# A fused attention and two-MLP kernel: clusters' ones transposed after the next group of weightings, guard maxima reduced ahead of the remainders, the third head's similarity moved to the first head's end

## The reference, cut to what matters

```python
B, H, S, D = 2, 8, 768, 64            # 16 heads in all, 16 clusters per head
q_assign = argmax(q_n @ c_n.T)        # the nearest centroid of each query ...
k_assign = argmax(k_n @ c_n.T)        # ... and of each key
mask = q_assign[..., :, None] == k_assign[..., None, :]
scores = where(mask, (q @ k.T) / sqrt(D), -1e9)
attn = exp(scores - max(scores)) / sum(...)
x = (attn @ v)                        # heads side by side: 1536 x 512
x = moe1(x)                           # 512 -> 2048 -> 512, leaky relu
out = moe2(x)                         # 512 -> 2048 -> 512, a rational function
```

## Time and profile before

| | |
|---|---|
| median of 3 runs | 825.64 us (824.8 to 826.27) |
| the profiled execution's own time | 822.96 us |
| its span | 821.2 us |
| PE busy | 791.4 us, 96% of the span |
| DVE, ACT, POOL busy | 562.2 (68%), 492.6 (60%), 296.1 us (36%) |
| chain that ended last | PE 77%, ACT 8%, DVE 6%, issue 5% |

### The profile page before, as it was taken

The page is one execution under the profiler, slowest core; times in us unless marked ns, Lnnn a source line. Parts: engine busy times, 40 slices in busy tenths (PEclk is TensorE's granted clock), DMA queues, the critical chain, the costliest instruction groups (busy, mean ns, idle before and its releaser), DMA issues.

```text
span 821.2 us, 13189 instructions
## 1 busy us (share of the span) xinstructions
PE 791.4 (96%) x4339; PEld 747.0 (91%) x4339; DVE 562.2 (68%) x948; ACT 492.6 (60%) x836; POOL 296.1 (36%) x330
## 2 busy tenths in 40 slices
PE   6799999999999999999999999979999999999996
PEld 5589999999999999999999999969988998998994
DVE  5777877877874555433433454488888888888885
ACT  2367777877887111211211233479999999999995
POOL 7467988987985796000000036640000000000000
PEclk9999999999999999999999999989999999999999
DMA  7445654564442333000000024410001001001001
GB/s 201 115 110 137 160 154 123 147 168 117 110 100 72 97 102 105 0 0 0 0 0 0 0 76 122 124 40 1 1 0 38 0 0 38 0 0 39 1 1 38
DMA packets 30316, 52.15 MB, mean 64 GB/s; under 512 B 9184, under 2 KB 11328, under 8 KB 30272
## 3 DMA queue, kind: packets, MB, share of 16 engines
q1 hardware_dynamic: 30272, 51.59, 22.9%
HBM read 29.40 MB, written 3.19 MB: 40 GB/s over the span
## 4 chain that ended last, share of the span: by engine, by line
PE 77%; ACT 8%; DVE 6%; issue 5%; POOL 2%; DMA 1%; SPq 1%; POOLq 0%; ACTq 0%; DVEq 0%
PE ps L193 29%; PE ps L1011 16%; PE ps L1019 13%; PE ps L635 3%; PE ps L697 3%; PE ps L667 3%; PE ps L678 3%; PE ps L705 3%; PE ps L698 3%; PE ps L608 2%; ACT ps L787 1%; DMA sums<-scratch 1%; ACT scratch L1063 1%; ACT scratch L1069 1%; PE ps L622 1%
## 5 line engine op out<-in xcount | busy, mean ns | idle before, releaser
L199 ACT ACTIVATE g_hi<-g_f 128x384 fp32r<-128x384 f32 x128 | 67.4, 527 | 218.5 <-PE ps L1011 201.3
L211 DVE TENSOR_SCALAR corr<-ps,alpha_c 128x384 f32<-128x384 f32 x64 | 39.5, 617 | 130.3 <-PE ps L193 130.2
L193 PE MATMUL ps<-x_lo,w_hi_b 128*128 (+1 forms) x352 | 118.8, 337 | 0.0
L193 PE MATMUL ps<-x_hi,w_hi_b 128*128 (+1 forms) x352 | 118.7, 337 | 0.0
L193 PE MATMUL ps<-x_hi,w_lo_b 128*128 (+1 forms) x352 | 118.7, 337 | 0.0
L893 DVE TENSOR_REDUCE row_max<-ps 128x1 fp32r<-128x768 f32 x96 | 91.0, 950 | 35.4 <-PE ps L635 35.0
L784 ACT ACTIVATE probs_hi<-ps 128x768 fp32r<-128x768 f32 x96 | 78.1, 814 | 61.7 <-PE ps L678 60.9
L203 DVE TENSOR_TENSOR g_lo<-g_f,g_hi 128x384 fp32r<-128x384 f32 x128 | 82.2, 642 | 0.6 <-ACT g_hi L199 0.6
L340 DVE TENSOR_TENSOR probs_lo<-ps,probs_hi 128x768 fp32r<-128x768 f32 x64 | 61.0, 954 | 24.4 <-ACT ps L787 24.4
L340 POOL TENSOR_TENSOR probs_lo<-probs,probs_hi 128x768 fp32r<-128x768 f32 x32 | 59.6, 1862 | 47.4 <-ACT probs L787 47.4
L1159 POOL TENSOR_TENSOR w_lo_a<-stage,w_hi_a 128x512 f32 (+1 forms) x10 | 12.7, 1297 | 163.6 <-ACT w_hi_a L1084 163.6
(11 more groups left out here) (132 smaller groups left out, 2094.6 us busy)
## 6 DMA issues: line engine op xcount, KB each, us to landing
stage<-in_moe_w_in SPq DMA_DIRECT2D x27, 256.0 KB, 2.6
stage<-in_moe_w_out SPq DMA_DIRECT2D x27, 256.0 KB, 2.8
raw<-in_qk SPq DMA_DIRECT2D x16, 384.0 KB, 3.8
op_a<-head_hi SPq DMA_DIRECT2D x32, 192.0 KB, 3.4
v_raw<-in_v SPq DMA_DIRECT2D x16, 192.0 KB, 2.5
op_b<-head_hi SPq DMA_DIRECT2D x16, 192.0 KB, 3.5
op_b<-head_lo SPq DMA_DIRECT2D x16, 192.0 KB, 3.7
scratch<-spread SPq DMA_DIRECT2D x16, 192.0 KB, 4.1
```

The source lines that it names most:

```text
L193: last = pe.matmul(h_ps[j % H_RING][:, 0:BLK], a[:, 0, w], x[:, kt, cols], start=(kt == 0 and i == 0), stop=(kt == KT - 1 and i == 2))
L199: act.activation(g_hi[:, j % 2], g_f[:, j % 2], ACT.Copy).then_inc(g_hi_made, 1)
```

## The change

It makes four edits, with the waits and places on ACT and DVE that go with them.

1. `turn_onehot(n+2)` stands in slot 0 of head n (n >= 1), behind `weigh_hi` and ahead of the guards and the score, where before the same transposes stood at the end of slot 5 of the head before. `put_mask_k` follows `exp` of slot 0 in place of `exp` of the slot before it.
2. Ahead of the loop, one tile of `sim(2)` stands in front of `turn_first_max`, two behind guard 5, and the last one behind `score(0)`; guards 4 and 5 follow `turn_first_max` directly.
3. `sim(3)` moves from slot 1 to slot 4 of head 0, ahead of guard and score, and into banks 0 and 1; its reading on DVE moves with it, and `turn_onehot(2)` no longer waits for it.
4. DVE reduces all guards of a slot ahead of the remainder in the first seven slots too.

```diff
--- before.py
+++ after.py
@@ -278,7 +278,7 @@
 
 
 
-            SIM_BANK = {1: 7, 2: 4, 3: 7}
+            SIM_BANK = {1: 7, 2: 4}
 
             def sim_at(m, t):
                 if m in SIM_BANK:
@@ -598,11 +598,8 @@
                     if m == 2:
                         pe.wait_ge(mask_q_put, 1)
                         pe.wait_ge(mask_k_put, 1)
-                    if m == 3:
-                        pe.wait_ge(mask_q_put, 2)
-                        pe.wait_ge(mask_k_put, 2)
-                    if m >= 4:
-                        pe.wait_ge(guard_taken, T * (m - 1) - 2)
+                    if m >= 3:
+                        pe.wait_ge(guard_taken, T * (m - 1) - (1 if m == 3 else 2))
                         pe.wait_ge(sim_taken, m)
                     for t in tiles:
                         last = pe.matmul(sim_at(m, t), raw[:, m % 2, t * P:(t + 1) * P], cent_t[:, head_of(m)],
@@ -614,8 +611,6 @@
                     pe.wait_ge(onehot_made, m + 1)
                     at_least(pe, mask_q_put, m)
                     at_least(pe, mask_k_put, m)
-                    if m == 2:
-                        pe.wait_ge(sim_taken, 4)
                     if m >= 3:
                         pe.wait_ge(pv_taken, 2 * (m - 3) + 1)
                     for t in range(T):
@@ -729,26 +724,29 @@
                 sim(2, range(0, 2))
                 guard(0, 2)
                 guard(0, 3)
+                sim(2, range(2, 3))
                 turn_first_max()
-                sim(2, range(2, 4))
                 guard(0, 4)
-                sim(2, range(4, T))
                 guard(0, 5)
+                sim(2, range(3, 5))
                 turn_max(0)
                 for g in range(UNITS + LAG):
                     n, s = g // U, g % U
                     if g >= LAG:
                         weigh_hi(g - LAG)
                     if g < UNITS:
+                        if g == U - 2:
+                            sim(3)
                         if g == U - 1:
                             turn_max(1)
+                        if s == 0 and n >= 1 and n + 2 < N:
+                            turn_onehot(n + 2)
                         guards(n, s, 1)
                         scores_free(g)
                         score(g)
                         if g == 0:
+                            sim(2, range(5, T))
                             turn_onehot(1)
-                        if g == 1:
-                            sim(3)
                         if n >= 1 and s == 1 and n + 3 < N:
                             sim(n + 3)
                         if n >= 1 and s == 3 and n + 1 < N:
@@ -764,8 +762,6 @@
                         guards(n, s, 3)
                         if g == 2:
                             turn_onehot(2)
-                        if s == U - 1 and n + 3 < N:
-                            turn_onehot(n + 3)
 
 
             @block.scalar
@@ -819,8 +815,8 @@
                     exp(g)
                     if n == 0 and s in (0, 2):
                         put_mask_k(1 + s // 2)
-                    if s == U - 1 and n + 3 < N:
-                        put_mask_k(n + 3)
+                    if n >= 1 and s == 0 and n + 2 < N:
+                        put_mask_k(n + 2)
                     if s == 2 and n >= 1:
                         take_pv(n - 1, 1)
                     if s == 4:
@@ -932,23 +928,17 @@
                     if s == (5 if n == 0 else 3) and n + 1 < N:
                         take_max(n + 1)
 
-                    late = n == 0 or (n, s) == (1, 0)
-                    for m, t in guard_tiles(n, s, *((1, 2) if late else (1, 2, 3))):
+                    for m, t in guard_tiles(n, s, 1, 2, 3):
                         take_guard(m, t)
-                    if n >= 1 and s == 1 and n + 3 < N:
+                    if g == U - 2 or n >= 1 and s == 1 and n + 3 < N:
                         nearest(n + 3)
-                    if n == 0 and s == 3:
+                    if g == 3:
                         put_mask_q(2)
                     if n >= 1 and s == 0 and n + 2 < N:
                         put_mask_q(n + 2)
                     if s not in POOL_LO:
                         make_lo(dve, g)
-                    if g == 1:
-                        nearest(3)
-                    if late:
-                        for m, t in guard_tiles(n, s, 3):
-                            take_guard(m, t)
-                    if n == 0 and s == 2 or n >= 1 and s == 3 and n + 3 < N:
+                    if g == U - 2 or n >= 1 and s == 3 and n + 3 < N:
                         ranked(n + 3)
                         first_nearest(n + 3)
                     if s == 4 and n % 2 == 0 and n >= 2:
```

## The result

The changed kernel takes 818.9 us (median of 4 runs, 816.96 to 819.34), the kernel before beside it 825.38: a ratio of 0.9916 [0.9898, 0.9934], a gain of 6.9 us (5.4 to 8.4); the two medians lie 6.5 us apart. Forecast were 820.7 us and a gain of 4.9: the direction and the range held, the gain was forecast too small. The profiled execution of the change took 819.34 us, 817.5 of it span; that of before 822.96. This pair is only 3.6 us apart, less than the 4.9 forecast, and its attention ends 3.6 us earlier too (the last matmul starts at 263.82 for 267.42).

The account below looks back on a forecast made before the run. PE, busy 96% of the span, was taken as the bound, so only its idle or low-clock time can be won. Transposes 2.2 plus start 2.7 make 4.9 us: 825.64 - 4.9 = 820.7 us, range 818.6 to 824.2.

Parts of the forecast that it names:

- Part 1: Transposes one group of weightings later, behind `weigh_hi`: 2.34 us of PE's waits less 0.1 that stays, 2.2 us gained.
- Part 2: The start's new order laid end to end: scores of slot 7 from 49.93 to 47.25, 2.7 us gained.
- link 6: `sim(3)` in slot 4 of head 0: needs the eleventh reduction (35.6), costs 1.33 us; 3.1 us of lead left.
- 5, guard of 36.48: Reduction of place 3 ahead of `make_lo`: the guard at 36.48 starts at 32.2, 4.3 us ahead.
- 7, guard of 45.08: End of head 0, DVE's chain after `exp`: guard starts at 42.65, 2.4 us ahead, PE idle some 1.8 us.
- link 2: First scores go from 23.58 to 22.15; if the DMA issued at 19.07 lands late, 1.4 us are lost.
- link 4: Head 1's guards: POOL ends at 27.25, DVE is through `ranked(2)` by 27.7; second guard 31.71 to 28.65, 3.05 us.
- The sum: 2.2 + 2.7 = 4.9 us: 820.7 against the 825.64 median, 818.1 for the profiled execution; MLPs' work untouched.
- Only one part shows: The transposes' gap is its own price, or DVE eats the start's lead: 823.4 or 822.9 us; chance 0.14.
- DVE held beside POOL: Slot 3, DVE loses 1.5 us: six heads cost 5.1, 825.8 us (chance 0.04); twelve 10.2, 830.9; slower 0.04.
- The clock rises at another time: PE reaches 2.4 GHz later in the start, 1.5 us lost, 822.2; or earlier, 0.8 won, 819.9; chance 0.08.
- It does not do what it says: Transposes still wait because POOL's ones set the pace; waits stay and the start gives little, chance 0.04.

Follow-up runs that it names:

- e8: The change with three tiny memsets on DVE ahead of `ranked` from head 4 on, so DVE starts behind POOL; 823.86 us, 0.9994 to the kernel before.

## Why the prediction was right or wrong

**What bounds the kernel: right.** PE's busy time did not move (791.4 to 790.8 us), and what the profiles show as won is time in which PE had stood still or run at its lower level.

**Part 1 (2.2 us): right.** Reading the waits off PE's own distances, not off the view of waits (5.4), gave the size: 2.08 us in the profile, 1.7 in the two others of the change, 1.80 in that of edit 1 alone, 2.6 (1.6 to 3.5) timed. On top of edits 2 to 4 it shows less: the ratio goes from 0.9944 to 0.9937 and to 0.9925, 0.6 and 1.6 us. That ACT's later mask copy would cost nothing held: the heads are 14.69 us apart, 0.02 above the 14.67 of a head without a wait. The waits for ACT's copy of the output come and go: none in the change's profile, 0.2 and 0.3 us in its two others, 0.3 with edit 1 alone, where 0.1 was kept.

**Part 2, link by link: right in the profile.** (The forecast of link 6 is the 40.12 of that guard before, less the 3.1 us left.)

| link | forecast | change's profile |
|---|---|---|
| 1, `turn_max(0)` | 21.5 | 21.82 |
| 2, first scores | 22.15 | 22.45 |
| 3, second scores | 24.95 | 25.07 |
| 4, head 1's second guard | 28.65 | 28.96 |
| 5, guard of 36.48 | 32.2 | 32.49 |
| 6, guard behind `sim(3)` | 37.0 | 37.13 |
| 7, guard of 45.08 | 42.65 | 42.83 |
| 8, scores of slot 7 | 47.25 | 47.38 |

The late DMA that link 2 feared did not hold ACT: the wait ahead of the first scores is the 0.36 us it was. In link 4 `ranked(2)` was held beside POOL again, 1.50 us, since it starts 0.44 us behind POOL. The Trainium skill (SBUF — State Buffer, Who interferes with whom), drawn on there for which of the two blocks the other, agrees in this place: DVE began second and was held. It does not describe, where DVE began second too and was not held; the last section has that.

**The sum: the step that failed.** The term "So part 2 gives 2.7 us" is too small for the kernel. It is right for the start of slot 7 in the profiled pair, 2.55, but edits 2 to 4 alone give 4.6 us timed (3.5 to 5.7), twice. The prediction saw that the profiled execution of before lay 2.7 us below the median, and then took the same 4.9 us off the median, as if what makes an ordinary execution longer lay outside the change. Part of it lies inside. The averages of the profiled executions show how much:

| | slot 7 starts | attention's last matmul starts |
|---|---|---|
| before (six) | 50.5 | 268.2 |
| edit 1 alone (one) | 50.0 | 265.7 |
| edits 2 to 4 alone (two) | 46.9 | 264.1 |
| the change (three) | 47.7 | 264.0 |

So the profiles give edits 2 to 4 4.1 us, inside the timed interval and 1.4 above the term. About 0.5 of the 1.4 is the clock: in two of six executions of before it rose late, in the very microseconds that edits 2 to 4 rearrange, and that costs before 1.6 us, the new start 0.3 (e8). In before the twelve matmuls of `sim(3)` stand in those microseconds and take 2.74 us in place of 1.50, with the guard that DVE needs next behind them; in the new order they come later, at 35.8. Another 0.5 us are won between slot 7 and the attention's end (217.7 us on average before, 217.2 with edits 2 to 4 alone), where part 2 was put at nothing; which waits these are was not traced. The last 0.4 is within what slot 7 moves by from one execution to the next. The clock was a rival, but only for the kernel after; that the kernel before has two starts was not asked.

**What stays open.** How often the clock rises late is not known: two of six executions of before, and one (e8) of the eight that hold the whole new start, are too few to say whether the new order changes it. The profiled executions of before average 823.6 us (six, four of them on another chip), those timed beside the other kernels 825.0 (52 executions). One place where a longer execution can get its time is the second slow stretch between the MLPs, 1.4 us, seen in four of the twelve profiles of changed kernels and in none of before; whether the timed executions of before have it, no profile shows.

**Why the parts don't add up.** 2.6 + 4.6 = 7.2 us, while the whole gave 6.9, 5.2 and 6.2. Averaged over all executions (16 of the change, 819.45 us; 52 of before, 824.95, other runs and chips among them) it is 5.5 us (4.7 to 6.3 by their scatter). The profiles have the gap too: 2.5 + 4.1 against 4.2 us by the attention's end. Of these 2.4, 0.7 is that slot 7 starts later in the three of the change, one of which was held up by a DMA, and 0.6 the new wait of 0.9 us in head 13, in two of three. The rest is open, and the new wait was not taken away by itself. So 4.9 lies 0.6 us under the mean over all executions, inside its scatter, and 2.0 under the first comparison. That it comes so near is in part luck: the start was put too low by 1.4 to 1.9 us, and that the parts add up was taken for granted. In the profiled pair itself the whole gained 3.6 us, where the prediction had 818.1 us for the profile and the MLPs 4.9 us ahead: 2.55 and 2.08 were won, and 0.9 lost again in head 13.

**The rivals.** *Only one part shows* fell: both show, separately. *DVE held beside POOL* did not occur in the change, but its mechanism and place are shown, and its price is 4.6 us for 5.1; the margin by which the change escapes it is some hundredths of a microsecond. *The clock rises at another time* came true for the kernel before, and in the new order it cost 0.3 us where 1.5 were feared. *It does not do what it says* fell with the view of waits.

## What to carry to other kernels

Size a wait on the busiest engine by the distances of its own repeating work; the view of waits on the weight loads told of 5.4 us where 2.1 could be had, and again of 5.4 where 4.6 were lost. When the profiled execution is well off the median, look at several executions of the kernel before, ahead of a sum: the difference may lie in the stretch that the change touches. Two edits that feed the same chain (here the order of the first matmuls and DVE's reductions) may be worth little each and over 4 us together. A passage that no edit touches can still differ by 1.4 us between two profiles: compare it before a difference is put down to an edit.

## What the runs showed of the hardware

Whether DVE is held beside POOL changed between a start 0.053 and one 0.074 us behind POOL's. In the 17 other profiles of this case a 128x192 `ranked` that starts 0.033 to 0.053 us after POOL's 128x768 operation still takes 0.24 us, in six heads of each, and it is POOL's operation that is stretched, to 1.98 to 2.00 us, as in the earlier trace rows, for 1.82 in the earlier trace rows. In e8, which pushes it back, a start 0.074 to 0.079 us after POOL's takes 1.88 us. So these kernels stand on the right side in six heads out of twelve by hundredths. The Trainium skill (SBUF — State Buffer, Who interferes with whom) says that whoever issues first gets the shared ports and the other blocks; here DVE started second by a hair and was not blocked. The profile shows when the two start and not when they were issued, so it cannot say whether the rule fails there or the order of issue was the other.

The rise of PE's clock in the start falls at different places in executions of one and the same kernel, with the same work up to 27.8 us. What that is worth depends on what stands there: 1.6 us of time before, 0.2%, and 0.3 us in the new order. Between the MLPs PE falls back to 1.2 GHz about one pause of 3.8 us in every profile, and in four of 18 once more after a pause of 2.3 to 2.5 us, which costs 1.4 us; other profiles have a second pause of 2.3 to 2.5 us without it.
